# Three engines get a new order of their instructions in a fused attention and MLP kernel

## The reference

```python
# q, k, v: (4 batches, 8 heads, 576 tokens, 64), float32; top_k = 32
scores = matmul(q, k.T) / 8
kth    = np.partition(scores, -top_k, axis=-1)[..., -top_k:-top_k + 1]
scores = where(scores >= kth, scores, -1e9)
attn   = exp(scores - max(scores)); attn = attn / (sum(attn) + 1e-9)
x = matmul(attn, v)                       # then (4*576 = 2304 tokens, 8*64 = 512)
x = ((1 / (1 + exp(-(x @ w_gate)))) * (x @ w_val)) @ w_out      # 512 -> 1536 -> 512
h = maximum(x @ w_in, 0); out = (h * h) @ w_out2                # 512 -> 2048 -> 512
```

## Time and profile before

| | |
|---|---|
| median of 3 runs | 1199.86 us (1199.26 to 1201.14) |
| the profiled execution | 1199.26 us |
| its span (first to last instruction) | 1197.5 us |
| mean granted TensorE clock | 0.989 |
| busy: PE, DVE, ACT, POOL | 96%, 71%, 62%, 52% |
| chain that ended last: PE, ACT, POOL, DVE | 86%, 5%, 3%, 3% |
| matmul lines | L569 chunk 0; L583, L584, L585 chunks 1 to 5; L485, L501, L524 attention |

### The profile page before, as it was taken

How to read it: one execution, slowest core, us unless ns; L and a number is a source line. 1 busy time by engine, 2 the same in 40 slices (tenths; PEclk the granted TensorE clock), 3 DMA queues, 4 the chain that set the end, 5 groups by cost and what they waited for, 6 DMA issues and landing times.

```text
span 1197.5 us, 21823 instructions
## 1 busy us (share of the span) xinstructions
PE 1153.3 (96%) x7520; PEld 998.8 (83%) x7520; DVE 846.7 (71%) x1756; ACT 739.2 (62%) x1758; POOL 626.9 (52%) x539
## 2 busy tenths in 40 slices
PE   4589999999999999999999999999999999999999
PEld 2468889999889999899877777777878888899998
DVE  7999888787997888999677679974766676001130
ACT  6887788776876776787666657755554466111130
POOL 5886677776775554665444436653444356012130
PEclk9779999999999999999999999999999999999999
DMA  9988777888769666757645455555554544577774
GB/s 362 336 290 288 240 249 250 301 286 294 266 221 338 218 209 213 237 192 231 220 154 179 158 188 193 199 176 193 184 167 158 169 151 167 197 246 254 255 252 141
DMA packets 90397, 270.13 MB, mean 226 GB/s; under 512 B 10032, under 2 KB 16176, under 8 KB 90288
## 3 DMA queue, kind: packets, MB, share of 16 engines
q1 hardware_dynamic: 90288, 268.74, 66.7%
HBM read 228.33 MB, written 40.37 MB: 224 GB/s over the span
## 4 chain that ended last, share of the span: by engine, by line
PE 86%; ACT 5%; POOL 3%; DVE 3%; issue 3%; DMA 0%; ACTq 0%; SPq 0%; POOLq 0%; DVEq 0%
PE ps L583 21%; PE ps L585 20%; PE ps L584 20%; PE ps L569 7%; PE ps L524 7%; PE ps L485 6%; PE ps L501 5%; DVE work L770 1%; DVE top L768 1%; POOL below L837 1%; ACT scores L617 1%; ACT below L622 1%; POOL full_buf L877 1%; ACT probs L636 1%; POOL probs L842 0%
## 5 line engine op out<-in xcount | busy, mean ns | idle before, releaser
L837 POOL TENSOR_TENSOR below<-scores,below 128x576 f32<-128x576 f32 x144 | 206.2, 1432 | 290.7 <-ACT below L629 288.6
L768 DVE MAX8 top<-work 128x8 f32<-128x576 f32 x432 | 312.3, 750 | 0.5
L583 PE MATMUL ps<-xy_hi,ring 128*128 128x512 f32 (+2 forms) x800 | 289.0, 361 | 0.0
L585 PE MATMUL ps<-xy_hi,ring 128*128 128x512 f32 (+2 forms) x800 | 281.6, 352 | 0.0
L584 PE MATMUL ps<-xy_lo,ring 128*128 128x512 f32 (+2 forms) x800 | 281.1, 351 | 0.0
L770 DVE MATCH_REPLACE8 work<-top,work 128x576 f32<-128x576 f32 x288 | 213.8, 742 | 0.0
L583 PE MATMUL ps<-g_hi,ring 128*128 128x384 f32 (+2 forms) x560 | 201.7, 360 | 2.8 <-DVE g_lo L805 2.8
L585 PE MATMUL ps<-g_hi,ring 128*128 128x384 f32 (+2 forms) x560 | 197.1, 352 | 0.0
L584 PE MATMUL ps<-g_lo,ring 128*128 128x384 f32 (+2 forms) x560 | 196.7, 351 | 0.0
L583 PEld LDWEIGHTS ps<-xy_hi,ring 128*128 128x128 f32 x800 | 150.2, 188 | 18.5 <-issue 6.7
L585 PEld LDWEIGHTS ps<-xy_hi,ring 128*128 128x128 f32 x800 | 150.1, 188 | 13.2
(11 more groups left out here) (58 smaller groups left out, 1761.3 us busy)
## 6 DMA issues: line engine op xcount, KB each, us to landing
ring<-w_split SPq DMA_DIRECT2D x318, 512.0 KB, 3.8
wring<-w_in SPq DMA_DIRECT2D x113, 256.0 KB, 4.6
w_split<-stage SPq DMA_DIRECT2D x46, 512.0 KB, 4.3
w_split<-ring SPq DMA_DIRECT2D x22, 512.0 KB, 5.2
vt<-v_in SPq DMA_DIRECT2D x16, 480.0 KB, 4.8
heads_in<-qk_in SPq DMA_DIRECT2D x16, 336.0 KB, 4.5
vt<-v_in SPq DMA_DIRECT2D x16, 320.0 KB, 3.3
heads_in<-qk_in SPq DMA_DIRECT2D x16, 304.0 KB, 4.7
```

The lines of the kernel that those rows point to most:

```text
L583: nc.tensor.matmul(dst, w_hi, hi[:, k, 0:WIDTH[c]], start=first, stop=False)
L585: mm = nc.tensor.matmul(dst, w_lo, hi[:, k, 0:WIDTH[c]], start=False, stop=final)
L768: nc.vector.max(out=best, in_=sc if step == 0 else wk).then_inc(sel_step[t % 2], 1)
L837: nc.gpsimd.tensor_tensor(out=below[:, t % 2, :], in0=scores[:, t % PLACES, :], in1=below[:, t % 2, :], op=ALU.subtract).then_inc(mask_don ...
```

## The change

Nothing is computed differently, and PE's own order is the same. The change moves work in the other engines' programs.

- ACT, slots from 15 on: evac of the part [2] before comes ahead of `copy_pt`, and evac [0] comes behind `split_x` and `exp`.
- ACT, slots before 15: `copy_x` comes ahead of `copy_scores`, and `exp` and `copy_pt` ahead of the splits of weights. The splits are placed one slot earlier (`SPLIT_AT`).
- DVE: select 0 and 1 come first, `invert` behind them, and evac [0] and [1] together behind select 2.
- POOL: `split_x` comes ahead of evac [0] and [1].
- `AHEAD` goes from 4 to 5 and `STORE_LAG` from 2 to 3. The split of a weight of chunk 1 is made one block earlier than before, and the stores of chunk 0 come one block later.

```diff
-AHEAD = 4
-STORE_LAG = 2
+AHEAD = 5
+STORE_LAG = 3
...
-    SPLIT_AT.setdefault(1 + _k * (MLP_AT[0] - 2) // NPRE, []).append(_k)
+    SPLIT_AT.setdefault(_k * (MLP_AT[0] - 1) // NPRE, []).append(_k)
...
 # ACT, slots before MLP_AT[0], behind find_below and enlarge
+                if s - 1 in PROD_AT:
+                    copy_x(PROD_AT[s - 1])
                 if s - 1 in SCORE_AT:
                     for t in tiles_of(SCORE_AT[s - 1]):
                         copy_scores(t)
                 last = s == MLP_AT[0] - 1
                 if last:
                     copy_pt(PROD_AT[s])
+                if 0 <= s - MASK:
+                    exp(s - MASK)
+                if s in PROD_AT and not last:
+                    copy_pt(PROD_AT[s])
                 for k in SPLIT_AT.get(s, []):
                     split_weights(k)
-                if s - 1 in PROD_AT:
-                    copy_x(PROD_AT[s - 1])
-                if 0 <= s - MASK:
-                    exp(s - MASK)
                 if last:
                     copy_x(PROD_AT[s])
-                if s in PROD_AT and not last:
-                    copy_pt(PROD_AT[s])
...
 # ACT, slots from MLP_AT[0] on, behind find_below and enlarge
+                for c, n in blocks_of(SHARES[s - 1][2]):
+                    evac(c, n)
                 if s in PROD_AT:
                     copy_pt(PROD_AT[s])
-                for c, n in blocks_of(SHARES[s - 1][2]):
-                    evac(c, n)
-                for c, n in blocks_of(SHARES[s][0]):
-                    evac(c, n)
                 for c, p in X_AT.get(s, []):
                     split_x(c, p)
                 if s - MASK < NT:
                     exp(s - MASK)
+                for c, n in blocks_of(SHARES[s][0]):
+                    evac(c, n)
...
 # DVE
             for s in range(SLOTS):
+                select_both(s, [0, 1])
                 if s in NORM_AT and s >= MLP_AT[0]:
                     invert(NORM_AT[s])
-                select_both(s, [0])
                 for c, n in blocks_of(SHARES[s - 1][2]) if s else []:
                     evac(c, n)
-                select_both(s, [1])
-                for c, n in blocks_of(SHARES[s][0]):
-                    evac(c, n)
                 select_both(s, [2])
-                for c, n in blocks_of(SHARES[s][1]):
-                    evac(c, n)
                 if s in NORM_AT and s < MLP_AT[0]:
                     invert(NORM_AT[s])
+                for c, n in blocks_of(SHARES[s][0] + SHARES[s][1]):
+                    evac(c, n)
                 select_both(s, [3])
...
 # POOL, behind normalise
-                for c, n in blocks_of(SHARES[s][0]):
-                    evac(c, n)
-                for c, n in blocks_of(SHARES[s][1]):
-                    evac(c, n)
                 for c, p in X_AT.get(s, []):
                     split_x(c, p)
+                for c, n in blocks_of(SHARES[s][0] + SHARES[s][1]):
+                    evac(c, n)
```

More of the change, by code:

```diff
@@ L601, in _ @@
                     times_v(PROD_AT[s])
-                for c, h in SHARES[s][1]:
-                    mlp_half(c, h)
-                for c, h in SHARES[s][2]:
+                for c, h in SHARES[s][1] + SHARES[s][2]:
                     mlp_half(c, h)
```

## The result

The changed kernel takes 1213.51 us, median of 5 runs (1212.88 to 1215.07), and the kernel before, run beside it, 1200.77 us. The ratio is 1.0111, with a 95% interval of 1.0096 to 1.0126: slower by 1.1%, some 13 us. The prediction had said slower, by 7 us, and at most 1212. The direction was right, the size was not. The profiled execution took 1213.16 us with a span of 1211.3 us, 13.8 us more than the span before.

A forecast was written before the change was run, and what follows sets the result against it. The prediction took DVE as the bound up to 85 us and PE from there on. Its terms, 1.8 + 0.4 + 1.3 + 2.0 + 0.7 + 2.0 − 1.2, gave +7.0 us, hence 1206.9 us as a median, range 1198 to 1212.

The forecast's parts named there:

- In front of 85 us: Prologue, where DVE was taken as the bound with unchanged order: nothing gained by ACT's new order, and no loss counted.
- A: Start of chunk 0: first gate's tanh, now behind exponential and sum, makes PE wait for its accumulator; +1.8 us, ends 0 and 3.
- the 0.6 us for slot 16: Slot 16: the next gate loses the cover of the mask's wait and falls behind by about 0.6 us.
- B: Chunk 0 and chunk 1's gate and y: copies to pt behind evacs +0.4 us, weight splits in front +1.3 us.
- C: Chunk 1's squares: late relu, delayed copies to pt and last low part cost +2.0 us; ends −2.8 and +5.
- the wait of 2.76 us: PE's wait before 349.99 for DVE's last low part, end of chunk 1's squares; expected to absorb PE's earlier losses.
- D: Last weight splits, near 363: needed a block earlier, they wait for slow loads; +0.7 us, ends 0 and 2.
- E: Chunk 2, slots 83 to 85: evac and relus delay copies to pt; +2.0 us, ends −1.5 and +3.
- F: Credit on ACT: evac of the part [2] before fills waits for transposes, so later work comes earlier; −1.2 us.
- rival 2: Faster: evacs in ACT's waits for transposes move its chain up and PE's 2.8 us wait goes; 1195.5 us, chance 0.16.
- Two signs: Forecast wrong if ACT's wait for transposes shrinks from 104 us and PE's 2.8 us wait goes with it.
- Rival 3: Chunk 1: all 16 DVE subtractions of L805 collide with POOL and take 1.53 instead of 0.78 us; 1215 us, chance 0.05.

The follow-up runs named there:

- the prologue's run alone: Kernel before with only ACT's new order ahead of slot 15 and the weight splits placed one slot earlier: 1205.2 us, ratio 1.0043.
- the run with the cover restored: Changed order on ACT ahead of slot 15 only, but weight splits ahead of `exp` again, against the kernel before: 1200.83 us, ratio 1.0003.
- the changed kernel with the old prologue: Changed kernel with ACT's order and the splits ahead of slot 15 as before the change, timed against the kernel before: 1209.04 us, ratio 1.0075.
- the run with that exchange alone: Kernel before with only evac of the part [2] before moved ahead of `copy_pt` on ACT, slots from 15 on: 1205.85 us, ratio 1.0044.
- the exponential first alone: Kernel before with only `split_x` and `exp` moved ahead of evac [0] on ACT, slots from 15 on: 1206.12 us, ratio 1.0049.
- the run with the splits last: Kernel before with `AHEAD = 5`, `STORE_LAG = 3` and chunk 1's weight splits behind the evac's own work on ACT and POOL: 1199.53 us, ratio 0.999.

## Why the prediction was wrong, step by step

**In front of 85 us: the step that failed.** "DVE's order is the same as before, [...] and ACT's new order there doesn't touch the bound: nothing gained." From DVE's 78.17 busy of 85 us the prediction concluded that nothing could be gained, and never asked what could be lost. It wrote itself that what can be lost has no such limit, and then applied that only behind 85 us. The loop of signs, mask, exponential, copies to pt and weight copies, all ACT's but the mask, became a bound of its own once the weight copies no longer ran beside POOL's mask, and PE and the first matmul of the MLP stand at its end. It put the stretch at nothing; it was worth +4.3 us, by the prologue's run alone and, with up to a microsecond open, by the run with the cover restored. Without it the forecast of +7.0 would stand against 13.9 − 4.3 = 9.6 us, within its range, as the changed kernel with the old prologue does at 1209.04. The prediction had no term for the clock either, though the earlier trace rows showed it at 0.84.

**A: right, too large.** +0.9 us where 1.8 was forecast. The mechanism is in the rows, wait and releaser as named. The first term alone was right (1.53 us of wait, less the 0.56 us that went); the 0.6 us for slot 16 didn't come.

**B: right as a sum.** +1.4 us for what was put at 0.4 + 1.3 = 1.7. POOL's low part behind the weight split shows as a wait of 0.53 us in front of 283.33, for the 0.7 forecast. That an evac ahead of pt costs in chunk 0 was wrong: the run with that exchange alone shows nothing up to 300 us. In the changed kernel chunk 0 behind its first blocks lost 0.1 us; the exponential first alone loses 1.2 us there.

**C: right in place, half the size.** Put at +2.0, and +0.7 for D in the same stretch; measured +4.8. The first relu's wait was right (1.20 us for 1.4). The copies to pt were named as held up by a high part that waits for POOL's square, and put at 0.3 to 1.0 us each; they cost 0.96, 2.41 and 0.96 us. The prediction then took most of it back, against the wait of 2.76 us. That one absorbed just its 2.76 us, once. And 1.7 us of PE's time at the lower clock were in no term; by the run with the old prologue, where the clock stays up, about 0.5 of them count.

**D: wrong mechanism.** Put at +0.7 for a late load; `AHEAD = 5` alone cost 3.0 us. ACT's weight copies did wait for loads, 3.7 us in 4 places in the changed kernel, but just as long (4.8 us) in the run with the splits last, which isn't slower than before. No copy waits near 363, where the prediction had it; the longest such wait is 1.6 us near 300. Where the split stands relative to the squares decides.

**E: right.** +2.4 us for 2.0. In slot 83 the second score tile now waits 1.15 us, where there was no wait, two slots later 0.84 instead of 0.35, and one relu block 0.24.

**F and rival 2: the credit didn't come.** Two signs that the prediction had named as speaking against it did appear: ACT's wait for transposes shrank, from 104.0 to 50.6 us, and the wait of 2.8 us went. They were poor signs. The first only moved to the mask's wait, and the second was paid for by earlier waits of PE. A wait of PE that vanishes while the same matmul starts 11.4 us later is no gain.

**Rival 3 fell**: the 16 subtractions together became shorter, not longer. What the Trainium skill says of the shared port pair ("SBUF — State Buffer", "Who interferes with whom") is not refuted by that; the trace of the kernel before agrees with it.

```profile
308.73 0.47 DVE L805 TENSOR_TENSOR g_lo<-full_buf,g_hi 128x320 fp32r<-128x320 f32 x1
308.81 1.67 POOL L837 TENSOR_TENSOR below<-scores,below 128x576 f32<-128x576 f32 x1
...
330.96 1.29 POOL L832 TENSOR_TENSOR ring<-wring,ring 128x512 fp32r<-128x512 f32 x1
...
331.07 1.53 DVE L805 TENSOR_TENSOR g_lo<-full_buf,g_hi 128x320 fp32r<-128x320 f32 x1
```

The first subtraction began ahead of POOL's operation and took 0.47 us, and POOL's took 1.67 instead of about 1.43. The second began 0.11 us behind POOL's, and ended 0.35 us after it. All 16 of this trace follow the pattern: the twelve that begin while POOL is working end about 0.35 us behind POOL's instruction, and the other four take 0.47 us. So what counts is how much of POOL's instruction is left when a subtraction begins, and the prediction took pairs to meet more of it without a row that shows it.

## What to carry to other kernels

An engine that is the bound in a stretch shows that nothing can be gained there by others, not that nothing can be lost: another engine, nearly as full and with a wait for a third in its program, is the second bound. When an instruction leaves another's wait, price both ends, the wait that opens and what the instruction now delays. And ahead of a just-in-time copy look first for an instruction that itself waits for a third engine: without one the evacs ahead of pt cost nothing up to 300 us, with one they cost waits of up to 3.46 us.

## What the runs showed that was not expected

The clock that the chip granted in the first 85 us was lower after: 0.76 against 0.84 before, means between its two levels of 1.2 and 2.4 GHz, with PE busy 49.37 and 50.10 us. From 28 to 78 us no instruction of PE stands in the chain that ended last, so the clock isn't what paid there: by then 3.4 of the prologue's 4.3 us are lost. The last 0.9 us come from 78.0 to 81.3 us, where PE works without a pause at the lower level; in the kernel before the clock was up again from 76.0 us on.

Behind 85 us the clock falls for 3.4 or 6.8 us in nine of the sixteen traces with a change, ten times in all, and not in the trace of the kernel before. Each time PE has waited for 2.4 to 3.5 us at that place or up to 1.6 us ahead of it. Not each such wait brings a fall: two of the traces with a wait of 2.7 to 2.8 us for the last low part have none. A fall of 3.4 us costs PE 1.4 to 1.7 us, which is also the distance between the three groups of the kernel before. So a wait of PE can cost more than it lasts. For the change as a whole this is little: of its six executions the one with the highest granted clock, 0.996, took 1212.88 us, and the profiled one, with 0.982, 1213.16.

Idle time of an engine off the critical path can shift from one wait to another by tens of microseconds (ACT: −53.4 us for transposes, +42.3 us for the mask) for a change of 1% in the time, so its size says little about what is to be won from it.
